# Opening of an attention-to-MLP kernel rewritten: four tiles transposed on TensorE, k-v moved behind the first MLP products, one excursion per tile

## The chip, the cores and the metric

One NeuronCore of one Trainium2 chip. The metric is the device time of one execution in microseconds; lower is better.

## The reference

A gated linear attention (r, k, v: 4 x 8 heads x 768 x 48), its output as 3072 rows of 384 features, and two MLPs behind it, all in float32.

```python
for t in range(S):
    kt, vt, rt = k[:, :, t], v[:, :, t], r[:, :, t]
    cur = einsum('bhd,bhe->bhde', u[None] * kt, vt)
    y[:, :, t] = einsum('bhd,bhde->bhe', rt, state + cur)
    state = w[None, :, :, None] * state + einsum('bhd,bhe->bhde', kt, vt)
h = x @ w_in;  g = relu(h) ** 2;     x = g @ w_out      # 384 -> 2048 -> 384
h = x @ w_in2; g = h - tanh(h);      x = g @ w_out2
```

## The kernel before

The sequence is cut into chunks of 128 positions; 4 batches x 6 chunks are 24 tiles, four tiles (TPB, one chunk of each batch) make a block of 512 rows, six blocks. A tile is loaded twice: "tt" holds r and k transposed (features on partitions), "nat" holds r, k, v with positions on partitions. Its steps: `decay` (DVE, L741) multiplies tt by powers of w; `products` (GpSimd, L316, L318) forms r k u, `bonus` (DVE, L747) sums it to one number per head, `diagonal` (ACT, L399) writes these as diagonal matrices; `score` (TensorE, L569) makes kT x rT, `mask` (DVE, L754) copies the causal half beside the diagonal; `attend` (TensorE, L583 for the state, L597 for v) makes the output, `x_high` (ACT, L407) and `x_low` (DVE, L780) split it into two fp32r parts; `decay_k` (GpSimd, L324) and the k-v product (TensorE, L605, the end of `attend`) feed `update_state` (DVE, L769 to L775).

The MLPs run in 96 steps each, m = 16 i + n: `first1(m)` is 9 products of 512 columns into hid, `act1` (DVE, L788, L790), `hi1` (ACT, L413) and `lo1` (GpSimd, L329) make the two parts of g, `second1(m)` is 9 products into acc. `first1` runs LAG = 3 steps ahead. Weights come in eight units per MLP; each is split by `split_hi` (ACT, L392) and `split_lo` (DVE, L799, or GpSimd, L335, for units 0 and 1). The raw units of MLP 1 lie in four stages that share their space with tiles; SP loads them in a written order (L260 to L282).

All engines run an order written out by hand, each waiting on counting semaphores. Tile T of blocks 1 to 5 is scored at n = 0, 3, 6, 9 of the block before and attended one step later (`scores_at`, `y_at`); `prepare_at` has its decay and bonus one step ahead of the scores. `stay_warm` multiplies the identity with itself. The second MLP has `poly_pick` (L847 to L858) in place of `act1`; its last three steps take the low part of g last (`second2_low_last`, L662, L663, L666).

## Time and profile before

| | us |
|---|---|
| median of 3 runs | 921.73 (920.44 to 923.01) |
| the profiled execution | 922.49 |
| its span, first to last instruction | 920.7 |

| stretch, us | PE busy | DVE busy | granted clock | DMA GB/s |
|---|---|---|---|---|
| 0 to 10 | 8.34 | 7.20 | 1.00 | 294 |
| 10 to 20 | 4.97 | 5.15 | 0.83 | 291 |
| 20 to 30 | 5.23 | 5.16 | 0.66 | 200 |
| 30 to 40 | 6.98 | 4.45 | 0.66 | 2 |
| 40 to 50 | 9.32 | 3.22 | 1.00 | 205 |
| 50 to 60 | 6.93 | 8.18 | 0.97 | 312 |
| 60 to 70 | 10.00 | 4.34 | 0.86 | 2 |
| 200 to 300 | 100.00 | 50.45 | 1.00 | 62 |

The first table tells the total, the second where TensorE is not filled. The granted clock is a share of full speed, so 0.5 is 1.2 GHz and 1.0 is 2.4 GHz; where TensorE stands, it says nothing of work. The first product of MLP 1 starts at 46 us.

### The profile page before, as it was taken

To read this page: it belongs to the slowest core of one execution; us is meant where nothing else is said; L and a number is where in the kernel's file an instruction comes from. 1 tells how busy PE (TensorE), PEld (TensorE's weight loads), DVE (VectorE), ACT (ScalarE), POOL (GpSimd) and SP (SyncE) were. 2 spreads that over 40 slices of the span, in tenths; PEclk is the share of its full clock that TensorE was granted. 3 is DMA by queue.
4 is the path that set the end of the run, shared out by engine and by line. 5 is a ranking of instruction groups with operands and counts; after the bars stand their busy time and mean duration, and the time that the engine had idled before them with its cause. 6 is when DMAs were issued, how large, how long until landed. Compare 5 with 4: busy or idle time off the path is not lost.

```text
span 920.7 us, 13868 instructions
## 1 busy us (share of the span) xinstructions
PE 896.6 (97%) x5340; PEld 736.9 (80%) x5340; DVE 591.2 (64%) x789; ACT 453.1 (49%) x852; POOL 477.1 (52%) x370
## 2 busy tenths in 40 slices
PE   5789999999999999999999999999999999999997
PEld 5668788888888888888888878888888888888886
DVE  6358736545563555445346668778787787787775
ACT  3333414222231322323124477777777777777774
POOL 5543434525443442433225776666666666666664
PEclk9799999999999999999999999999999999999999
DMA  6253111120311112020212200000000000000000
GB/s 254 107 206 140 53 54 54 58 103 1 106 54 54 53 54 106 1 92 16 103 35 69 68 1 1 35 1 1 34 1 1 35 1 0 36 1 1 35 0 35
DMA packets 12162, 47.49 MB, mean 52 GB/s; under 512 B 1472, under 2 KB 1600, under 8 KB 12096
## 3 DMA queue, kind: packets, MB, share of 16 engines
q1 hardware_dynamic: 12096, 46.60, 13.8%
q8 instruction: 42, 0.69, 0.3%
q14 instruction: 24, 0.20, 0.1%
HBM read 41.88 MB, written 4.72 MB: 51 GB/s over the span
## 4 chain that ended last, share of the span: by engine, by line
PE 82%; DVE 8%; POOL 4%; ACT 3%; issue 2%; DMA 1%; ACTq 0%; DVEq 0%; POOLq 0%
PE acc L551 13%; PE acc L553 12%; PE acc L552 12%; PE hid L551 9%; PE hid L552 9%; PE hid L553 9%; PE sc L552 3%; PE sc L553 3%; PE sc L551 3%; PE sc L569 2%; PE y L597 2%; PE sc L605 2%; PE y L583 2%; POOL area L340 1%; DVE area L847 1%
## 5 line engine op out<-in xcount | busy, mean ns | idle before, releaser
L329 POOL TENSOR_TENSOR g_l<-g_f,g_h 128x512 fp32r<-128x512 f32 x96 | 131.6, 1372 | 278.1 <-ACT g_h L413 278.1
L551 PE MATMUL acc<-g_h,wout_h 128*128 128x512 f32 x567 | 225.8, 398 | 0.6 <-POOL g_l L345 0.5
L553 PE MATMUL acc<-g_h,wout_l 128*128 128x512 f32 x567 | 221.9, 391 | 0.0
L552 PE MATMUL acc<-g_l,wout_h 128*128 128x512 f32 x567 | 221.4, 391 | 0.0
L413 ACT ACTIVATE g_h<-g_f 128x512 fp32r<-128x512 f32 x96 | 60.7, 632 | 315.8 <-DVE g_f L790 299.4
L340 POOL TENSOR_TENSOR area<-area 128x512 f32<-128x512 f32 x96 | 125.8, 1311 | 104.6 <-ACT area L431 104.6
L788 DVE TENSOR_SCALAR g_f<-hid 128x512 f32<-128x512 f32 x96 | 66.2, 690 | 164.4 <-PE hid L553 161.5
L551 PE MATMUL hid<-x_h,win_h 128*128 128x512 f32 x432 | 168.5, 390 | 1.2 <-DVE g_f L788 1.2
L552 PE MATMUL hid<-x_l,win_h 128*128 128x512 f32 x432 | 168.1, 389 | 0.0
L553 PE MATMUL hid<-x_h,win_l 128*128 128x512 f32 x432 | 168.0, 389 | 0.0
L345 POOL TENSOR_TENSOR g_l<-g_f,g_h 128x512 fp32r<-128x512 f32 x96 | 128.4, 1338 | 33.6 <-ACT g_h L446 33.6
L551 PEld LDWEIGHTS acc<-g_h,wout_h 128*128 128x128 f32 x567 | 106.7, 188 | 25.8 <-POOL g_l L345 1.5
L847 DVE TENSOR_SCALAR area<-area 128x512 f32<-128x512 f32 x96 | 88.3, 920 | 59.3 <-POOL area L340 59.3
L553 PEld LDWEIGHTS acc<-g_h,wout_l 128*128 128x128 f32 x567 | 106.8, 188 | 22.8
L552 PEld LDWEIGHTS acc<-g_l,wout_h 128*128 128x128 f32 x567 | 106.8, 188 | 21.0
L551 PEld LDWEIGHTS hid<-x_h,win_h 128*128 128x128 f32 x432 | 81.2, 188 | 18.7 <-DVE g_f L788 1.8
L553 PEld LDWEIGHTS hid<-x_h,win_l 128*128 128x128 f32 x432 | 81.1, 188 | 17.0
L552 PEld LDWEIGHTS hid<-x_l,win_h 128*128 128x128 f32 x432 | 81.2, 188 | 16.9
L853 DVE COPY_PREDICATED area<-area,y 128x512 f32<-128x512 uint32 x96 | 71.7, 747 | 3.3
L790 DVE TENSOR_TENSOR g_f<-g_f 128x512 f32<-128x512 f32 x96 | 70.9, 738 | 3.3
L399 ACT ACTIVATE area<-area,x2T 128x128 f32<-128x128 f32 x192 | 58.8, 389 | 28.8 <-DVE x2T L747 28.8
L439 ACT ACTIVATE area<-area 128x512 f32<-128x512 f32 x96 | 60.0, 625 | 19.4 <-POOL area L340 19.4
(110 smaller groups left out, 1169.7 us busy)
## 6 DMA issues: line engine op xcount, KB each, us to landing
x2T<-in_nat SPq DMA_DIRECT2D x13, 672.0 KB, 5.8
area<-in_nat SPq DMA_DIRECT2D x11, 672.0 KB, 4.9
x2T<-in_tt SPq DMA_DIRECT2D x12, 512.0 KB, 3.8
area<-in_tt SPq DMA_DIRECT2D x11, 512.0 KB, 3.6
out<-x2T SPq DMA_DIRECT2D x18, 256.0 KB, 2.2
x2T<-in_win SPq DMA_DIRECT2D x4, 768.0 KB, 7.7
x2T<-in_wout SPq DMA_DIRECT2D x4, 768.0 KB, 5.0
area<-in_win SPq DMA_DIRECT2D x4, 768.0 KB, 4.4
```

The source lines that it names most:

```text
L329: pool.tensor_tensor(g_l[:, m % 4, :], g_f[:, m % 2, :], g_h[:, m % 4, :].bitcast(F32), ALU.subtract).then_inc(s_gl1, 1)
L340: pool.tensor_tensor(ratio[m % 2], ratio[m % 2], sq[m % 2], ALU.mult).then_inc(s_pp, 1)
L345: pool.tensor_tensor(g_l[:, m % 4, :], g_f[:, m % 2, :], g_h[:, m % 4, :].bitcast(F32), ALU.subtract).then_inc(s_gl2, 1)
L413: act.activation(g_h[:, m % 4, :], g_f[:, m % 2, :], ACT.Copy).then_inc(s_gh1, 1)
L439: act.activation(ratio[m % 2], ratio[m % 2], ACT.Copy, scale=C5, bias=1.0).then_inc(s_ratio, 1)
L551: pe.matmul(dst, wh, xh, start=first, stop=False)
L552: pe.matmul(dst, wh, xl, start=False, stop=False)
L553: return pe.matmul(dst, wl, xh, start=False, stop=last)
L788: dve.tensor_scalar(g, hid1[m % 2], 0.0, None, ALU.max).then_inc(s_relu, 1)
L790: dve.tensor_tensor(g, g, g, ALU.mult).then_inc(s_g1, 1)
L847: dve.tensor_scalar(sq[m % 2], sq[m % 2], Q_SMALL, None, ALU.is_ge).then_inc(s_big, 1)
L853: dve.copy_predicated(tanh[m % 2], sq[m % 2].bitcast(U32), tanh_ps[:, :]).then_inc(s_sel, 1)
```

## The change

Tiles 0 to 3 come as nat alone; TensorE transposes their r and k (`transposed`), and DVE multiplies the result by the powers out of PSUM, in two halves. GpSimd does the four tiles' products first and then the whole split of unit 0, high part too. The powers of w are made with fewer waits, partly on ACT. K-v leaves `attend`: `key_value` runs behind attend(3) for tiles 0 and 2 and behind first1(0) for 1 and 3, as 16 products of 32 rows and 48 columns. The fillers are spread over the opening. From block 0 on, score(T + 1), attend(T) and key_value(T) stand together at n = 1, 4, 7, 10, score(4) alone at m = 0; decay and bonus of tile T + 2 follow one step later, and key_value(T) waits for mask(T + 1), whose scores share its bank. SP loads tiles 4 and 5 ahead of units 3 to 7 and tiles 6 and on behind them. Channel order in the weights is the natural one. At the end, first2(95) follows first2(94), and four steps take the low part last. Cut to its core, eight blanks of indentation less:

```diff
-NATW = C + H * HP + PAIRS * VW
-WARM_UP = 24
+RK = H * HP
+NATW = 2 * RK + PAIRS * VW
+WARM_UP = 6
...
+def prod_of(T):
+    if T < TPB:
+        return first_prod[:, C * (T % 2):C * (T % 2) + C].rearrange("p (h d) -> p h d", h=H)
+    return r_of(T)
...
+def decays(T):
+    return 2 * (T + 1) if T < TPB else TPB + T + 1
+KV_FIRST = [0, 2, 1, 3]
+def kv_count(T):
+    return KV_FIRST.index(T) + 1 if T < TPB else T + 1
+def kv_ps(T):
+    at = 512 * (T // 2) if T < TPB else 0
+    return sc_ps(T)[:, at:at + PAIRS * D]
...
+def slot_at(i, n):
+    return TPB * (i + 1) + n // 3 if 0 <= i < BLOCKS - 1 and n % 3 == 1 and 0 <= n < 12 else None
+def update_at(i, n):
+    return slot_at(i, n - 1)
+def diagonal_at(i, n):
+    T = slot_at(i, n + 1)
+    return T + 1 if T is not None and T + 1 < TILES else None
+def decay_k_at(i, n):
+    return slot_at(i, n + 1)
 def prepare_at(i, n):
-    if n == FT - 1:
-        return scores_at(i + 1, 0)
-    return scores_at(i, n + 1)
-def products_at(i, n):
-    if n >= FT - 2:
-        return scores_at(i + 1, 0) if n == FT - 2 else None
-    return scores_at(i, n + 2)
+    T = slot_at(i, n - 1)
+    if i == 0 and n == 0:
+        return TPB + 1
+    return T + 2 if T is not None and T + 2 < TILES else None
...
-        if n in (1, 5, 6, 7):
-            sp.wait_ge(*lo_done(0, {1: 0, 5: 1, 6: 2, 7: 3}[n]))
+        if n in (4, 5):
+            sp.wait_ge(s_kv, TPB)
+        elif n >= 2:
+            sp.wait_ge(*lo_done(0, {2: 0, 3: 1, 6: 2, 7: 3}[n]))
         at = STAGE1_AT[n]
         sp.dma_start(stage1[at], (wout1 if n % 2 else win1)[n // 2]).then_inc(s_stage1[at], 16)
     def load_tile(T):
-        before = T - 2 if T > 5 else T - 4
-        if before < LAST_KV:
-            sp.wait_ge(s_kv, before + 1)
+        before = T - 2
+        if before < TPB:
+            sp.wait_ge(s_sc, before + 1)
         else:
             sp.wait_ge(s_y, before + 1)
         load_tt(T)
+        if T < TPB + 2:
+            sp.wait_ge(s_kv, kv_count(T - TPB))
+        elif before < LAST_KV:
+            sp.wait_ge(s_kv, kv_count(before))
         load_nat(T)
...
-    load_tt(0)
     load_nat(0)
     sp.dma_start(u_all, u_rep).then_inc(s_u, 16)
-    load_tt(1)
-    load_nat(1)
+    for T in range(1, TPB):
+        load_nat(T)
     load_unit1(0)
-    load_nat(2)
-    load_tt(2)
-    load_nat(3)
-    load_tt(3)
     load_unit1(1)
-    load_tile(4)
-    sp.wait_ge(s_kv, TPB)
     load_unit1(2)
-    load_unit1(3)
-    load_unit1(4)
-    load_tile(5)
-    load_unit1(5)
-    load_unit1(6)
-    load_unit1(7)
+    load_tile(TPB)
+    load_tile(TPB + 1)
+    for n in range(3, UNITS):
+        load_unit1(n)
     for T in range(6, TILES):
         load_tile(T)
...
+    pool.memset(state_all, 0.0).then_inc(s_const, 1)
...
+        prod = prod_of(T)
+        if T < TPB:
+            after(pool, s_c, T - 1)
+        pool.tensor_tensor(prod, r, k, ALU.mult).then_inc(s_rk, 1)
         pool.wait_ge(s_rk, T + 1)
-        pool.tensor_tensor(r, r, u_all, ALU.mult).then_inc(s_ruk, 1)
+        pool.tensor_tensor(prod, prod, u_all.rearrange("p (h d) -> p h d", h=H), ALU.mult).then_inc(s_ruk, 1)
...
+        if T < TPB:
+            pool.wait_ge(s_tr, 2 * T + 2)
...
+    for T in range(TPB):
+        products(T)
+    pool.wait_ge(*landed(0, 0))
+    pool.tensor_copy(unit_parts(0)[0], unit_raw(0, 0)).then_inc(s_whi0, 1)
+    split_lo(0, 0)
     pool.wait_ge(s_tab, 1)
-    decay_k(0)
-    products(1)
-    decay_k(1)
-    split_lo(0, 0)
-    for T in range(2, TPB):
-        products(T)
-        decay_k(T)
+    decay_k(KV_FIRST[0])
+    decay_k(KV_FIRST[1])
+    decay_k(KV_FIRST[2])
+    decay_k(KV_FIRST[3])
     split_lo(0, 1)
...
-            T = prepare_at(i, n)
+            T = decay_k_at(i, n)
             if T is not None:
                 decay_k(T)
-            if i == 0 and n == 0:
-                decay_k(TPB)
-            T = products_at(i, n)
...
+    half = P // 2
+    act.wait_ge(s_setup, 14)
+    act.activation(pow_k[:, :, 0:half], pow_r[:, :, P - 1:half - 1:-1], ACT.Copy).then_inc(s_pow, 1)
+    act.wait_ge(s_setup, SETUP_DONE)
+    act.activation(pow_k[:, :, half:P], pow_r[:, :, half - 1::-1], ACT.Copy).then_inc(s_pow, 1)
+    for side in range(2):
+        rows = slice(HP * side, HP * side + D)
+        act.activation(dec_tile[rows, :, D * side:D * side + D],
+                       w_pow[rows, 7, :].unsqueeze(2).to_broadcast([D, PAIRS, D]), ACT.Copy).then_inc(s_tile, 1)
     act.wait_ge(s_powT, 1)
-    act.activation(dec_k, hid34[:, 0:512].rearrange("p (h e) -> p h e", h=H)[:, :, 0:D],
-                   ACT.Copy).then_inc(s_tab, 1)
+    act.activation(dec_k, acc2[:, :].rearrange("p (h e) -> p h e", h=H)[:, :, 0:D], ACT.Copy).then_inc(s_tab, 1)
     act.wait_ge(s_const, 3)
     diagonal(0)
     diagonal(1)
-    split_hi(0, 0)
+    diagonal(2)
     x_high(0)
-    diagonal(2)
+    diagonal(3)
     x_high(1)
-    diagonal(3)
     x_high(2)
+    x_high(3)
     split_hi(0, 1)
-    x_high(3)
     split_hi(0, 2)
...
+            if m == 0:
+                diagonal(TPB)
+            T = diagonal_at(i, n)
             if T is not None:
                 diagonal(T)
             if m + LAG < STEPS:
                 hi1(m + LAG)
-            T = y_at(i, n)
+            T = slot_at(i, n)
             if T is not None:
                 x_high(T)
...
-    def stay_warm(count):
+    def stay_warm(count, bank):
         for _ in range(count):
-            pe.matmul(hid34[:, 512:512 + P], ident, ident, start=True, stop=True)
+            pe.matmul(bank[:, 0:P], ident, ident, start=True, stop=True)
+    def transposed(T):
+        pe.wait_ge(s_nat[set_of(T)], 16)
+        rk = set_nat[set_of(T)][:, 0:2 * RK]
+        for half in range(2):
+            after(pe, s_dec, 2 * (T - 1) + half + 1)
+            for a in range(PAIRS):
+                at = 512 * half + P * a
+                mm = pe.transpose(hid34[:, at:at + P], rk[:, at:at + P], ident)
+            mm.then_inc(s_tr, 1)
     def score(T):
-        pe.wait_ge(s_dec, T + 1)
-        before = T - 1 if T < TPB else T
-        after(pe, s_scm, before)
-        after(pe, s_state, min(before, LAST_KV))
+        pe.wait_ge(s_dec, decays(T))
+        after(pe, s_scm, T - 1 if T < TPB else T)
+        if T >= TPB:
+            pe.wait_ge(s_state, min(T if T == TPB else T - 1, LAST_KV))
         rT, kT, dst = rT_of(T), kT_of(T), sc_ps(T)
         for a in range(PAIRS):
             for g in range(2):
         opened = [False] * 4
         after(pe, s_xl, T - 1 if T < TPB else T)
         if T >= TPB:
-            pe.wait_ge(s_state, T - 3)
+            pe.wait_ge(s_state, kv_count(T - TPB))
             for a in range(PAIRS):
                 for part in range(3):
                     c, quad = divmod(3 * a + part, 4)
         turns = [[], [], [], []]
         for a in range(PAIRS):
-            for part, at, head in ((0, 0, 0), (1, 32, 1), (2, 64, 0), (2, 80, 1)):
+            for part, at, head in ((0, 0, 0), (1, 32, 0), (1, 48, 1), (2, 80, 1)):
                 c, quad = divmod(3 * a + part, 4)
                 turns[quad].append((a, c, at, head))
         for turn in range(4):
                                skip_group_check=True)
                 opened[quad] = True
         mm.then_inc(s_y, 1)
-        if T < LAST_KV:
-            pe.wait_ge(s_kd, T + 1)
-            for a in range(PAIRS):
-                mm = pe.matmul(sc_ps(T)[:, VW * a:VW * a + VW], k_of(T)[:, P * a:P * a + P], v[:, a, :],
-                               start=True, stop=True)
-            mm.then_inc(s_kv, 1)
+    def key_value(T):
+        if T >= LAST_KV:
+            return
+        pe.wait_ge(s_scm, T + 1 if T < TPB else T + 2)
+        pe.wait_ge(s_kd, kv_count(T))
+        for a in range(PAIRS):
+            for quad in range(4):
+                at = HP * (quad // 2)
+                mm = pe.matmul(kv_ps(T)[32 * quad:32 * quad + 32, D * a:D * a + D],
+                               k_of(T)[:, P * a + 32 * quad:P * a + 32 * quad + 32],
+                               v_of(T)[:, a, at:at + D], start=True, stop=True)
+        mm.then_inc(s_kv, 1)
...
-    stay_warm(WARM_UP)
+    stay_warm(WARM_UP, hid34)
+    transposed(0)
+    stay_warm(4, y7)
     pe.wait_ge(s_pow, 2)
     for a in range(PAIRS):
-        mm = pe.transpose(hid34[:, P * a:P * a + P], pow_k[:, a, :], ident)
+        mm = pe.transpose(acc2[:, P * a:P * a + P], pow_k[:, a, :], ident)
     mm.then_inc(s_powT, 1)
+    stay_warm(4, y7)
     score(0)
+    transposed(1)
+    stay_warm(8, y7)
     score(1)
+    transposed(2)
+    stay_warm(8, y7)
+    transposed(3)
+    stay_warm(8, y7)
     attend(0)
     score(2)
+    pe.wait_ge(s_tab, 1)
+    stay_warm(8, acc2)
     attend(1)
     score(3)
+    stay_warm(8, hid34)
     attend(2)
-    stay_warm(8)
+    stay_warm(8, hid34)
     attend(3)
-    stay_warm(12)
+    key_value(KV_FIRST[0])
+    key_value(KV_FIRST[1])
     for m in range(LAG):
         first1(m)
+        if m == 0:
+            key_value(KV_FIRST[2])
+            key_value(KV_FIRST[3])
     for i in range(BLOCKS):
         for n in range(FT):
             m = FT * i + n
                 first1(m + LAG)
             else:
                 first2(m + LAG - STEPS)
-            if scores_at(i, n) is not None:
-                score(scores_at(i, n))
-            if y_at(i, n) is not None:
-                attend(y_at(i, n))
+            T = slot_at(i, n)
+            if m == 0:
+                score(TPB)
+            if T is not None:
+                if T + 1 < TILES:
+                    score(T + 1)
+                attend(T)
+                key_value(T)
             second1(m)
     for m in range(STEPS):
-        if m + LAG < STEPS:
+        if m + LAG < STEPS - 1:
             first2(m + LAG)
+            if m + LAG == STEPS - 2:
+                first2(STEPS - 1)
+        if m + LAG < STEPS - 1:
             second2(m)
         else:
             second2_low_last(m)
...
     def decay(T):
-        dve.wait_ge(s_tt[set_of(T)], 16 * loads_of(T))
-        both = set_tt[set_of(T)]
-        dve.tensor_tensor(both, both, dec_tt, ALU.mult).then_inc(s_dec, 1)
+        if T >= TPB:
+            dve.wait_ge(s_tt[T % 2], 16 * tt_loads(T))
+            dve.tensor_tensor(set_tt[T % 2], set_tt[T % 2], dec_tt, ALU.mult).then_inc(s_dec, 1)
+            return
+        after(dve, s_sc, T - 1)
+        for half in range(2):
+            at = slice(512 * half, 512 * half + 512)
+            dve.wait_ge(s_tr, 2 * T + half + 1)
+            if T == 0 and half == 1:
+                dve.wait_ge(s_pow, 2)
+            dve.tensor_tensor(set_tt[T % 2][:, at], hid34[:, at], dec_tt[:, at], ALU.mult).then_inc(s_dec, 1)
...
         dve.wait_ge(s_ruk, T + 1)
         after(dve, s_diag, T - 1)
-        dve.tensor_reduce(c_sum[T % 2], r_of(T).rearrange("p (h d) -> p h d", h=H), AX_X,
-                          ALU.add).then_inc(s_c, 1)
+        dve.tensor_reduce(c_sum[T % 2], prod_of(T), AX_X, ALU.add).then_inc(s_c, 1)
...
+        for g in range(2):
+            rows, cols = slice(HP * g, HP * g + HP), slice(D * g, D * g + D)
+            kv = kv_ps(T)[rows, :].rearrange("p (a e) -> p a e", a=PAIRS)
+            if T < TPB:
+                ins = dve.tensor_tensor(st[rows, :, cols], kv, dec_tile[rows, :, cols], ALU.mult)
+            else:
+                ins = dve.tensor_tensor(st[rows, :, cols], kv, st[rows, :, cols], ALU.add)
+            ins.then_inc(s_state if T < TPB and g == 1 else s_sum, 1)
...
+    half = P // 2
+    dve.memset(dec_tile, 0.0).then_inc(s_setup, 1)
+    dve.memset(pow_r[:, :, half:half + 1], 1.0).then_inc(s_setup, 1)
     dve.wait_ge(s_w, 16)
-    for i in range(7):
-        link(dve.tensor_tensor(w_pow[:, i + 1, :], w_pow[:, i, :], w_pow[:, i, :], ALU.mult))
-    link(dve.reciprocal(pow_r[:, :, 0], w_pow[:, 6, :]))
-    for i in range(7):
+    for i in range(6):
         e = 1 << i
-        step = w_pow[:, i, :].unsqueeze(2).to_broadcast([P, PAIRS, e])
-        link(dve.tensor_tensor(pow_r[:, :, e:2 * e], pow_r[:, :, 0:e], step, ALU.mult))
-    dve.tensor_copy(pow_k, pow_r[:, :, ::-1]).then_inc(s_pow, 2)
-    dve.wait_ge(s_pow, 2)
+        dve.wait_ge(s_setup, 2 * i + 2)
+        dve.tensor_tensor(pow_r[:, :, half + e:half + 2 * e], pow_r[:, :, half:half + e],
+                          w_pow[:, i, :].unsqueeze(2).to_broadcast([P, PAIRS, e]),
+                          ALU.mult).then_inc(s_setup, 1)
+        squared(i)
+    dve.wait_ge(s_setup, 14)
+    dve.reciprocal(w_pow[:, 8, :], w_pow[:, 6, :]).then_inc(s_setup, 1)
+    squared(6)
+    dve.wait_ge(s_setup, 16)
+    dve.tensor_tensor(pow_r[:, :, 0:half], pow_r[:, :, half:P],
+                      w_pow[:, 8, :].unsqueeze(2).to_broadcast([P, PAIRS, half]), ALU.mult).then_inc(s_setup, 1)
+    dve.wait_ge(s_setup, SETUP_DONE)
     decay(0)
-    for side, at, width in ((0, 0, 32), (1, 32, 32), (0, 64, 16), (1, 80, 16)):
-        rows = slice(HP * side, HP * side + D)
-        link(dve.tensor_copy(dec_tile[rows, :, at:at + width],
-                             w_pow[rows, 7, :].unsqueeze(2).to_broadcast([D, PAIRS, width])))
-    dve.wait_ge(s_const, 4)
     bonus(0)
     decay(1)
-    mask(0)
     bonus(1)
-    update_state(0)
-    x_low(0)
-    mask(1)
     decay(2)
     bonus(2)
-    update_state(1)
+    dve.wait_ge(s_const, 4)
+    mask(0)
+    bonus(3)
+    decay(3)
+    mask(1)
+    x_low(0)
+    mask(2)
     x_low(1)
-    mask(2)
-    decay(3)
-    bonus(3)
-    update_state(2)
+    mask(3)
     x_low(2)
-    mask(3)
-    update_state(3)
     x_low(3)
+    dve.wait_ge(s_const, 5)
+    update_state(KV_FIRST[0])
+    act1(0)
+    update_state(KV_FIRST[1])
+    update_state(KV_FIRST[2])
+    act1(1)
+    update_state(KV_FIRST[3])
+    act1(2)
     split_lo(0, 2)
-    for m in range(LAG):
-        act1(m)
     decay(TPB)
     bonus(TPB)
...
-            T = x_low_at(i, n)
+            T = update_at(i, n)
+            if T is not None:
+                update_state(T)
+            T = slot_at(i, n)
+            if T is not None and T + 1 < TILES:
+                mask(T + 1)
+            if m + LAG < STEPS:
+                act1(m + LAG)
+            if m == 0:
+                mask(TPB)
             if T is not None:
                 x_low(T)
-                update_state(T)
-            if m + LAG < STEPS:
-                act1(m + LAG)
-            T = scores_at(i, n)
-            if T is not None:
-                mask(T)
             T = prepare_at(i, n)
             if T is not None:
                 decay(T)
```

## Rows read from the trace of the kernel before

**Rows 1.** The page, part 1: engine busy us (share of the span) xinstructions.
```profile
PE 896.6 (97%) x5340; PEld 736.9 (80%) x5340; DVE 591.2 (64%) x789; ACT 453.1 (49%) x852; POOL 477.1 (52%) x370
```

**Rows 2.** Timeline, one tile in the steady state: start, us, engine, line, what.
```profile
157.78 0.39 PE L553 MATMUL hid<-x_h,win_l 128*128 128x512 f32 x1
...
158.10 0.97 PEld L569 LDWEIGHTS sc<-area 64*128 64x128 f32 x16 [0.35 <-issue]
...
159.53 0.39 PE L552 MATMUL acc<-g_l,wout_h 128*128 128x512 f32 x1
...
163.19 0.39 PE L553 MATMUL hid<-x_h,win_l 128*128 128x512 f32 x1
...
163.50 0.59 PEld L583 LDWEIGHTS y<-area 128*32 128x32 f32 x24 [0.35 <-issue]
...
165.17 0.97 PEld L605 LDWEIGHTS sc<-area 128*128 128x128 f32 x8 [0.20 <-issue]
...
166.40 0.39 PE L552 MATMUL acc<-g_l,wout_h 128*128 128x512 f32 x1
```

**Rows 3.** Timeline of TensorE in the opening.
```profile
1.66 7.09 PE L558 MATMUL hid<-area 128*128 128x128 f32 x48 [1.66 <-POOL area L305]
...
24.32 1.78 PEld L569 LDWEIGHTS sc<-x2T 64*128 64x128 f32 x16 [5.53 <-DVE x2T L741]
...
43.36 2.76 PEld L558 LDWEIGHTS hid<-area 128*128 128x128 f32 x24
...
46.06 0.48 PE L551 MATMUL hid<-x_h,win_h 128*128 128x512 f32 x1
```

**Rows 4.** Windows: us; busy PE, PEld, DVE, ACT, POOL; granted clock; DMA share, GB/s.
```profile
24.00:26.00 2.00, 1.68 (x16) 1.68 (x16) 0.26 (x1) 0.00 (x0) 1.92 (x2) 0.50 0.88 246
...
60.00:61.00 1.00, 1.00 (x4) 0.71 (x4) 0.61 (x2) 1.00 (x4) 0.00 (x0) 0.50 0.00 0
```

**Rows 5.** Timeline of TensorE behind the opening.
```profile
57.88 0.97 PEld L569 LDWEIGHTS sc<-x2T 64*128 64x128 f32 x16 [2.33 <-DVE x2T L741]
```

**Rows 6.** Timeline, first GpSimd product and first decay.
```profile
6.47 1.23 DVE L741 TENSOR_TENSOR x2T<-x2T,area 128x1024 f32<-128x1024 f32 x1
...
7.15 1.40 POOL L316 TENSOR_TENSOR x2T<-x2T 128x384 f32<-128x384 f32 x1 [5.30 <-DMA area<-in_u_rep]
```

**Rows 7.** Timeline of SP, and the DMA view of 70 to 80 us (us to landing).
```profile
71.07 0.33 SPq L249 DMA_DIRECT2D x2T<-in_wout  x1
...
71.92 0.43 SPq L243 DMA_DIRECT2D x2T<-in_nat  x1
...
x2T<-in_nat SPq DMA_DIRECT2D x1, 672.0 KB, 6.4
```

**Rows 8.** Timeline of 57 to 69 us: steps of a tile and of a unit.
```profile
57.74 0.55 DVE L747 TENSOR_REDUCE x2T<-x2T 128x8 f32<-128x384 f32 x1
...
58.32 2.45 ACT L399 ACTIVATE area<-area,x2T 128x128 f32<-128x128 f32 x8 [0.97 <-DVE x2T L747]
...
60.87 1.34 DVE L754 COPY_PREDICATED area<-x2T,sc 128x1024 f32<-128x1024 uint32 x1 [0.39 <-ACT area L399]
...
66.98 0.47 ACT L407 ACTIVATE x_h<-y 128x384 fp32r<-128x384 f32 x1
...
67.35 1.48 ACT L392 ACTIVATE wout_h<-x2T 128x1536 fp32r<-128x1536 f32 x1
...
68.86 2.18 DVE L799 TENSOR_TENSOR wout_l<-x2T,wout_h 128x1536 fp32r<-128x1536 f32 x1 [2.45 <-ACT wout_h L392]
```

**Rows 9.** The page, part 5: busy us, mean ns of one, idle before.
```profile
L788 DVE TENSOR_SCALAR g_f<-hid 128x512 f32<-128x512 f32 x96 | 66.2, 690 | 164.4 <-PE hid L553 161.5
...
L413 ACT ACTIVATE g_h<-g_f 128x512 fp32r<-128x512 f32 x96 | 60.7, 632 | 315.8 <-DVE g_f L790 299.4
```

**Rows 10.** Line L318 by source: duration ns min/median/max.
```profile
L318 POOL TENSOR_TENSOR x2T<-x2T,area x13: 995/1005/2400, 8.6 to 407.1; 128x384 f32<-128x384 f32 x13
```

**Rows 11.** Timeline of TensorE, last step.
```profile
914.37 0.50 PE L662 MATMUL acc<-g_h,wout_h 128*128 128x512 f32 x1 [0.90 <-ACT g_h L446]
```

103 lines of the change are left out of this document (40 added, 63 removed).

## The prediction

> **What bounds the kernel now.** I read the page first [rows 1]: TensorE is busy for 97% of the span, so outside the opening only work taken off TensorE, or a wait of TensorE removed, can move the time. The steady state is seen in the timeline of one tile [rows 2]: the matrix products follow each other every 0.227 us, 18 to a step, 4.09 us. Into this stream come two excursions per tile. The scores delay it from the product at 157.78 to the second one at 159.53: 1.75 less two intervals of 0.227, 1.30 us. Attention and k-v delay it from 163.19 to 166.40: 2.76 us. Together 4.05 us for a tile.
>
> The opening is different. The first MLP product starts at 46.04 us [rows 3]; up to there TensorE mostly waits for DVE or runs at half clock: the 16 score instructions that load in 0.97 us at 158.10 [rows 2] take 1.78 us at 24.32 [rows 3], and the clock view has 0.50 there [rows 4]. After 46 us TensorE loses little: 1.9 us (the weight loads 2.33) ahead of 57.88 on the decay of tile 4 [rows 5], and part of 59 to 63 us, where the granted clock is 0.50 (1.2 of 2.4 GHz) although the engine is busy [rows 4]; what it did before is that wait for tile 4 and a shorter one ahead of it. The change therefore has 46 us of opening to win from, some 5 us of stalls behind it, and 20 pairs of excursions.
>
> **The new opening.** The four 512 KB tile loads of transposed r and k go, so the natural tile 0 comes first. The old u_rep landed at 7.1 us [rows 6] with 1.36 MB queued up to and with it; three loads of 1.95 MB land 7.2 us after the issue of the first (71.07 to 71.92 plus 6.4) [rows 7]. By the slope between the two, about 0.45 MB per us, 0.75 MB issued at 1.2 us land near 5.5 us. From there TensorE has a nearly gapless list. Fillers: 56, at 2.76 us for 12 [rows 3], 12.9 us. Transposes, not in the old trace but for four: 36, 0.115 us each by the rows of the same 128-column shape, 4.2 us (from below half of it, from above 0.21 at half clock). Scores: 4 x 1.09 [rows 2]. Attention: 4 x 1.1, from the part of 163.50 to 165.17 that has no state product. K-v of two tiles: 1.9 us. Sum 27.7 us. The old start took 7.09 us for 24 fillers against 5.5 at the later rate [rows 3], so a cold start costs 1.6 us; I add 1.7. The first MLP product comes at F = 35.0 us, 11 us earlier. DVE's chain beside this list is shorter: from attend(1) to attend(3) it is a diagonal 2.45, x_high 0.47, x_low 0.55, mask 1.34 [rows 8], 4.9 us, against 5.9 us of TensorE's list; the two multiplies of a half tile are hidden behind fillers. The DVE set-up, whose last step gave way to decay(0) at 6.47 us [rows 6], has fewer waits between its steps and part of it moves to ACT; I take it under tile 0's landing and transposes. GpSimd has the four products (8 us), the new copy of unit 0 (estimate 1.7 us as half of a two-input 3.4, up to 3.5), its low part and four decays: done by about 27 us, under the 33 at which k-v wants them. The state memset lies under the wait for DMA. If that cover goes, each us is a us of F. Bounds for F: 33.5 (no cold part) to 38.
>
> **Behind the opening: what is late next.** I follow the written order of each engine, in us after F. TensorE: first1(0) 2.05, k-v of tiles 1 and 3 1.9, first1(1) and (2) 4.1, done at 8.2. DVE now puts act1(2) (0.69 + 0.7 [rows 9]) ahead of split_lo(0,2) (2.18) and that ahead of decay(4) (1.23) [rows 6, 8]: decay(4) ends at 13.0, while TensorE, after first1(3), wants it at 10.2. Stall 2.9, where the old one was 1.9. Then tile 4 and tile 5 are prepared one after the other, each a bonus 0.55, a diagonal 2.45, a mask 1.34 and between them a decay 1.23 [rows 6, 8]: mask(5) ends at 23.1.
>
> Here the new wait bites: key_value(T) writes the bank in which score(T+1) has just been put, so it waits for mask(T+1), and second1 and everything behind it queue behind that wait. For tile 4 TensorE stands 1.9 us. For tile 5 it is worse. SP has units 3 to 7 ahead of the loads of tile 6, and unit 7 waits for split_lo(0,3). That ends after mask(5) by act1(4) 1.4, hi1 0.65, x_high 0.45, split_hi(0,3) 1.48 and split_lo 2.18 [rows 8, 9]: at 29.2. Unit 7, tt 6 and nat 6 then land 7.4 us later [rows 7], at 36.6. The old order needed tile 6 only at step 5; the new one needs it at step 2. GpSimd's products 2.1 [rows 10] (38.7), bonus 0.6, diagonal 2.45, hi1(6) 0.65, split_hi(0,4) 1.45, split_lo(0,4) 2.2, which DVE has ahead of the mask, and mask(6) 1.4 end at 47.5. TensorE has 16.1 us of work from mask(5) on (k-v, three second1, three first1, score(6), attend(5)) and stands at 39.2. Stall 8.3 us. Whatever else TensorE loses before it is absorbed by it.
>
> From F + 47.5 to the start of the second block's steps I count k-v 1.0, second1 2.05, 11 steps of 4.09 and two excursions of 3.81: 55.7 us; the clock that falls in so long a wait costs 2 us more (the part of 59 to 63 us at half clock [rows 4], some 3.4 us, cost 1.7). Units 4 to 7 and tiles 7 and 8 come in time in this count, unit 6 by 1 us only. Sum 35.0 + 47.5 + 57.7 = 140.2 us. The old trace has 139.6 there (the score at 141.75 less a first1 of 2.05 and the gap). So the 11 us of opening are given back, +0.6.
>
> **The merged excursion.** From the last product to the score load 0.32, score 1.09 with its drain, attention 1.47, k-v, switch 0.20, re-entry 0.34, less 0.454 [rows 2]: 2.96 + k-v. K-v becomes 32 instructions with 48 columns instead of 8 with 112. None such is in the trace. The nearest are L583, 24 of the same tile shape in 0.59 us, 24.6 ns each, and the old k-v, 8 in 0.97, 0.12 us each. By columns alone (48 for 112) it could be 0.4, by the old row 0.97; I take 0.85, between L583's pitch (0.79) and the old row. That makes 3.81, 0.24 less than 4.05; even at 0.4 it would be 0.7 less. The wait for mask(T+1) takes some back: score's end 1.20 after its load, mask 1.37, hand-over 0.1, so 2.66, against attention's end at 2.56, and the re-entry after a wait 0.1. Left: 0.1 per tile with k-v, between -0.3 and 0.5. For tiles 8 to 19 it is 1.2 us, for 20 to 22, without k-v, 0.2 each, 0.6. Score(8) has already been done in block 0: 1.3.
> The row shows 24.6 ns with 128 columns in four column tiles. The Trainium skill, "TensorE: Matmul & The Clock Gate", section "Wait — 56ns, not 53.3ns?", says that start-to-start doesn't fall below about 25 ns however few the columns. By that 48 columns would gain nothing over 128: k-v 0.8, not 0.4, and the excursion stays near my value.
>
> **The tail.** first2(95) moves ahead of second2(91) and one more step takes its low part last. TensorE's last wait, 0.9 us at 914.37 on ACT's g_h [rows 11], goes: with the hidden product 2 us earlier, the chain of poly and pick ends under second2's products. -1.0, between -1.3 and +0.3.
>
> **Sum.** 920.7 + 0.6 - 1.2 - 0.6 - 1.3 - 1.0 = 917.2 us of span, 3.5 less; the profiled execution took 922.49 with 920.7 of span, the median of the runs is 921.73, and I apply the difference to that: 918.2 us. 0.3%, about what a measurement can tell from no change here, is 2.8 us, so the border to "faster" is 918.96.
>
> **Rivals.**
> (A) The 8.3 us stall doesn't come, because tile 6 lands or is masked in time. Against it stand the SP order and the split_lo in front of the mask. It would give 918.2 - 8.3 - 2 = 907.9. Chance 0.15.
> (B) The chain to mask(6) is longer than my minimum durations: one GpSimd product has 2.40 us against 1.0 [rows 10], and DVE and GpSimd work side by side here. 3 to 4 us more on it go one to one into the time: 921.7, no change. Chance 0.20.
> (C) Slower. The half clock stays through the opening. The old half clock at 24.32 followed a wait of TensorE of 5.5 us [rows 3, 4]; the new opening fills such gaps, but 36 of its instructions are transposes, whose effect on the clock no row shows. If they don't hold it, 16 us of the list at half clock bring 8 us more: F = 43 and 926.2 us. It decides from 13 us of half clock on (6.3 us more, over 924.5). Chance 0.12.
> The Trainium skill, "TensorE: Matmul & The Clock Gate", section "Part 4: PE-mode transpose", states that transpose mode doesn't engage the full clock in the way that a matmul does; that is the rule by which (C) would come out.
> The forecast itself has 0.53. Its own range is 914.5 to 922.5: F -1.5/+3, chain 2, excursions 2 to 3, tail 1, not all at once. It lies below 918.96 with some six tenths of its weight. Faster: 0.53 x 0.62 + 0.15, with a little for a shorter stall, 0.50. Slower 0.12 + 0.01. Same 0.37. The range, 911 to 925, leaves out most of (A) and (C).
>
> **What would show it.** First MLP product at 33.5 to 38 us. TensorE idle 2 to 3 us ahead of score(4), about 2 ahead of the k-v of tile 4, and 6 to 10 us ahead of that of tile 5, released by DVE's mask, with the nat 6 load landing some 37 us after F. Granted clock 1.00 through most of 10 to 35 us. Excursions of 3.8 to 4.0 us for score, attention and k-v together, k-v loads of 0.8 to 0.9. No wait on ACT's g_h in the last step. Wrong it would be if the second block began well before 136 us (A), or if k-v waited for the mask by more than 0.3 us in every tile, which over 15 tiles costs 4 us.

## The result, and the profile after

The changed kernel takes 909.63 us (median of 4 runs, 908.87 to 911.24) against 921.60 (4 runs, 920.44 to 923.01): a ratio of 0.9872, with the interval 0.9852 to 0.9891. It is faster by 12.0 us. The forecast was 918.2, and 909.63 lies below its range. The profiled execution took 909.35 us with a span of 907.4, where before had 920.7; 13.3 us of span are to be placed.

The page first, part 1 and the row of granted clock in part 2 (the latter in 40 slices of 22.7 us, tenths of full speed):

```profile
PE 886.2 (98%) x5888; PEld 733.9 (81%) x5888; DVE 596.4 (66%) x789; ACT 451.6 (50%) x855; POOL 490.6 (54%) x372
...
PEclk9987999999999999999999999999999999999999
```

TensorE is busy for 886.2 us instead of 896.6 [rows 1]. Of the 13.3 us, 10.4 are time in which it worked: work that it no longer does, or does in less time. The forecast gave the excursions only 3.1 us. The two slices below 9 in the clock row (45 to 91 us) are places to look at for waits.

The opening, in the timeline of TensorE (start, us, engine, line, what; in brackets the idle time before it and who ended it), and the windows over it (busy PE, PEld, DVE, ACT, POOL; granted clock; DMA share, GB/s):

```profile
5.65 0.85 PEld L610 LDWEIGHTS hid<-area,x2T 128*128 128x128 f32 x8 [1.35 <-DMA x2T<-in_nat]
...
32.81 0.50 PE L593 MATMUL hid<-x_h,win_h 128*128 128x512 f32 x1 [0.51 <-DVE x_l L863]
```

```profile
10.00:30.00 20.00, 20.00 (x263) 18.56 (x262) 11.72 (x16) 9.97 (x32) 13.39 (x11) 1.00 0.45 164
```

Tile 0 loads its first transposes at 5.65 us (5.5 was forecast), TensorE is busy without a gap from 10 to 30 us at granted clock 1.00, where the old opening had 0.50 at 24 us [rows 4], and the first MLP product comes at 32.81 us against 46.06 [rows 3]. So the opening alone is 13.2 us shorter.

What comes behind it, in the timeline of DVE, GpSimd and TensorE around the scores of tile 4:

```profile
45.61 2.28 DVE L817 TENSOR_TENSOR x2T<-x2T,area 128x1024 f32<-128x1024 f32 x1
...
46.77 1.98 POOL L355 TENSOR_TENSOR x2T<-x2T,area 128x384 f32<-128x384 f32 x1
...
47.94 2.08 PE L622 MATMUL sc<-x2T 64*128 64x128 f32 x16 [5.63 <-DVE x2T L817]
```

TensorE waits 5.63 us for decay(4). Before, the same wait was 1.91 us on the product (2.33 on the weight load [rows 5]), and 2.9 was forecast. The granted clock behind it is 0.50 from 48 to 52 us. Then the chain to mask(6), in the timeline of SP, GpSimd, DVE, ACT and TensorE from 63 to 82 us, and the windows behind it:

```profile
63.78 0.33 SPq L280 DMA_DIRECT2D x2T<-in_wout  x1
...
64.63 0.44 SPq L272 DMA_DIRECT2D x2T<-in_nat  x1
...
71.14 1.00 POOL L345 TENSOR_TENSOR x2T<-x2T 128x384 f32<-128x384 f32 x1 [9.55 <-DMA x2T<-in_nat]
...
73.86 2.45 ACT L432 ACTIVATE area<-area,x2T 128x128 f32<-128x128 f32 x8 [6.74 <-DVE x2T L831]
...
76.73 1.47 ACT L425 ACTIVATE win_h<-x2T 128x1536 fp32r<-128x1536 f32 x1
...
78.23 1.76 DVE L882 TENSOR_TENSOR win_l<-x2T,win_h 128x1536 fp32r<-128x1536 f32 x1 [2.26 <-ACT win_h L425]
79.91 1.28 DVE L837 COPY_PREDICATED area<-x2T,sc 128x1024 f32<-128x1024 uint32 x1
...
81.24 0.68 PEld L664 LDWEIGHTS sc<-area 128*32 128x32 f32 x32 [7.40 <-DVE area L837]
81.25 0.87 PE L664 MATMUL sc<-area 128*32 128x48 f32 x32 [7.13 <-DVE area L837]
```

```profile
81.00:85.00 4.00, 3.75 (x39) 3.06 (x40) 2.07 (x5) 2.38 (x3) 1.29 (x1) 0.50 0.45 132
85.00:88.00 3.00, 3.00 (x10) 2.35 (x10) 2.93 (x4) 0.00 (x0) 1.75 (x2) 0.65 0.18 75
88.00:92.00 4.00, 4.00 (x19) 3.31 (x18) 2.98 (x4) 0.77 (x2) 1.91 (x2) 1.00 0.02 4
```

This is the forecast chain link by link. SP sends unit 7 only when split_lo(0,3) is done, tile 6's nat behind it lands 6.5 us later and lets GpSimd begin at 71.14; bonus, diagonal, split_hi, split_lo and mask follow, and k-v of tile 5, which has to wait for mask(6), starts at 81.25 after TensorE has stood for 7.13 us. The clock is then 0.50 (1.2 GHz) up to 87 us, where the products come 0.43 us apart instead of 0.23, and 1.00 from 88.

The steady state, one tile, in the timeline of TensorE and DVE (the first line is the first product of the second block's steps):

```profile
138.88 0.39 PE L593 MATMUL hid<-x_h,win_h 128*128 128x512 f32 x1
...
144.78 0.39 PE L595 MATMUL hid<-x_h,win_l 128*128 128x512 f32 x1
145.09 0.97 PEld L622 LDWEIGHTS sc<-area 64*128 64x128 f32 x16 [0.35 <-issue]
...
146.30 1.36 DVE L837 COPY_PREDICATED area<-x2T,sc 128x1024 f32<-128x1024 uint32 x1 [3.76 <-PE sc L622]
146.76 0.89 PEld L650 LDWEIGHTS y<-area,x2T 128*32 128x32 f32 x32
...
147.72 0.41 PEld L664 LDWEIGHTS sc<-x2T 128*32 128x32 f32 x32
...
148.20 0.19 PEld L593 LDWEIGHTS acc<-g_h,wout_h 128*128 128x128 f32 x1
...
148.54 0.39 PE L594 MATMUL acc<-g_l,wout_h 128*128 128x512 f32 x1
...
160.67 1.16 PE L622 MATMUL sc<-x2T 64*128 64x128 f32 x16
```

These rows answer to [rows 2]. From the product at 144.78 to the second one behind the excursion at 148.54 are 3.76 us, less two intervals of 0.227: 3.31 us, where before had 4.05 in two parts. K-v's 32 instructions load in 0.41 us, and from its start to the next weight load at 148.20 are 0.48 us. DVE's mask ends at 147.66, and k-v starts at 147.72. Ahead of the second block one more k-v waits for its mask, that of tile 7, by 0.54 us at 115.81; behind it none does by more than 0.3 us. The period of a tile, 145.09 to 160.67, is 15.58 us; before it was 174.46 less 158.10, 16.36 (the next scores in the old trace start at 174.46). That is 0.78 us per tile.

The end, in the timeline of TensorE, the first product of each of the last two steps:

```profile
899.15 0.39 PE L722 MATMUL acc<-g_h,wout_h 128*128 128x512 f32 x1
...
901.19 0.39 PE L722 MATMUL acc<-g_h,wout_h 128*128 128x512 f32 x1
```

They stand 2.04 us apart and the last doesn't wait, where before the last one waited 0.90 us [rows 11].

The account, by the two places where the traces can be laid over each other. The steps of the second block start at 138.88 us against 139.61: 0.7 us earlier, although the opening had won 13.2. From there to the end of the span it is 768.5 us against 781.1: 12.6 us. Of these, twelve tiles at 0.78 are 9.4; 1.1 is the tail; 1.3 is the score of tile 8, which is now done in the first block and so is moved, not saved. Tiles 20 to 22 have no k-v: their scores stand 15.22 us apart (381.06, 396.28, 411.50), where the old trace has 15.47 (402.49, 417.96, 433.42), which makes 0.8. Sum 12.6. So nearly all that the change brings comes from the excursions, and the opening, for which most of the diff was written, brings almost nothing.

### The profile page after: what moved, and what is told of

Its sections match the earlier page's. It is cut to its first block, busy times and chain, and to the rows that moved or that the text cites. A ratio compares the mean times of both kernels' runs of the same rounds, so it can differ in the third digit from the quotient of the medians.

```text
span 907.4 us, 14993 instructions
## 1 busy us (share of the span) xinstructions
PE 886.2 (98%) x5888; PEld 733.9 (81%) x5888; DVE 596.4 (66%) x789; ACT 451.6 (50%) x855; POOL 490.6 (54%) x372
## 4 chain that ended last, share of the span: by engine, by line
PE 89%; DVE 4%; ACT 2%; POOL 2%; issue 1%; DMA 1%; SPq 0%; ACTq 0%; DVEq 0%; POOLq 0%
PE acc L593 14%; PE acc L594 13%; PE acc L595 13%; PE hid L593 10%; PE hid L594 10%; PE hid L595 10%; PE sc L594 3%; PE sc L593 3%; PE sc L595 3%; PE sc L622 3%; PE y L650 2%; PE y L636 1%; DMA x2T<-in_nat 1%; PE y L600 1%; POOL wout_l L369 1%
## 5 line engine op out<-in xcount | busy, mean ns | idle before, releaser
L873 DVE TENSOR_TENSOR g_f<-g_f 128x512 f32<-128x512 f32 x96 | 80.3, 837 | 3.3
```

What stands on the lines that cost most here:

```text
L873: dve.tensor_tensor(g, g, g, ALU.mult).then_inc(s_g1, 1)
```

## Experiments

Two theories stood against each other. Theory 1: k-v by 32 columns is much cheaper than the 0.85 us that I took, by columns rather than by instructions, and this carries the gain; the opening is given back to the wait for mask(6). Its rival: the gain is that of the merged excursion, or of the opening, and k-v's price isn't what counts. Each run below is the changed kernel with the edit shown; "over" and "under" are against its median of 909.63.

One thing is needed to read them. The opening itself doesn't take the same time in every execution (more under the hardware, below), and the four to ten runs of one kernel lie 1.3 to 3.2 us apart, in one case 4.7. A difference of one or two microseconds between two medians can be that. The traces separate it, since they show when the first MLP product starts (F), when the steps of the second block start, and what is left from there:

| trace | F | second block | between | to the end |
|---|---|---|---|---|
| before | 46.06 | 139.61 | 93.6 | 781.1 |
| changed | 32.81 | 138.88 | 106.1 | 768.5 |
| k-v wide | 33.45 | 139.58 | 106.1 | 774.9 |
| excursion apart | 32.79 | 136.48 | 103.7 | 771.9 |
| both undone | 36.01 | 141.07 | 105.1 | 778.5 |
| tile 6 early | 34.38 | 131.62 | 97.2 | 768.5 |
| tile 4 early | 35.21 | 138.64 | 103.4 | 768.5 |
| both, with split_lo moved | 34.81 | 131.73 | 96.9 | 768.6 |
| both, without that move | 34.71 | 130.07 | 95.4 | 768.7 |
| without 48 fillers | 31.19 | 137.18 | 106.0 | 768.5 |
| both early, without 48 fillers | 30.20 | 125.92 | 95.7 | 768.7 |
| old tail | 35.18 | 140.56 | 105.4 | 769.7 |

**K-v again as 4 products of 128 rows and 112 columns a tile, all else as changed.**

```diff
-for quad in range(4):
-    mm = pe.matmul(kv_ps(T)[32 * quad:32 * quad + 32, D * a:D * a + D], k_of(T)[:, P * a + 32 * quad:...], ...)
+mm = pe.matmul(kv_ps(T)[:, VW * a:VW * a + VW], k_of(T)[:, P * a:P * a + P], v_of(T)[:, a, :], ...)
```

> The changed kernel with one thing undone: k-v again as 4 products of 128 rows and 112 columns per tile in place of 16 of 32 rows and 48 columns. In the changed kernel's trace the 32 short instructions load in 0.41 us and the way back to the MLP product is 0.07 us, against 0.97 and 0.20 (inside the 1.09) in the old form. Theory 1 (my forecast missed because it priced k-v at 0.85 us plus a switch of 0.20): each tile from 6 to 19 costs 0.6 us more, 14 tiles 8.5 us, and the four k-v of the opening some 2 us, since the wait of tile 5 hangs on them: 8 to 11 us over the changed kernel, 918 to 920.5 us. Rival 2 (the gain is that of standing in one excursion, whatever k-v's form): not over 3 us, under 913 us.

Measured: 917.50 us (6 runs, 916.50 to 919.49), 0.9956 [0.9943, 0.9969]. It is 7.9 over. Its steady excursion, in the timeline of TensorE:

```profile
161.59 0.39 PE L595 MATMUL hid<-x_h,win_l 128*128 128x512 f32 x1
...
163.57 0.89 PEld L650 LDWEIGHTS y<-area 128*32 128x32 f32 x32
...
164.67 0.97 PEld L662 LDWEIGHTS sc<-area 128*128 128x128 f32 x8 [0.20 <-DVE area L834]
...
165.58 0.48 PE L593 MATMUL acc<-g_h,wout_h 128*128 128x512 f32 x1
...
165.90 0.39 PE L594 MATMUL acc<-g_l,wout_h 128*128 128x512 f32 x1
```

From 161.59 to 165.90 less 0.454 it is 3.86 us, 0.55 more than 3.31. K-v to the next product takes 0.91 instead of 0.48, and its start comes 1.10 us behind the start of L650's loads instead of 0.96. The row names the mask as what it waited for, but the old trace has the same 1.10 at that place (164.07 to 165.17), where k-v waits for no mask: going from column tiles of 32 into a whole array takes 0.14 us that the short form doesn't pay there. Twelve tiles at 0.54 (scores 16.12 us apart instead of 15.58) are the 6.4 us by which the trace is longer from the second block on; only 0.7 stands ahead of it, in F, so what the wide k-v of tiles 4 to 7 costs is hidden by the waits there. 917.50 is a little under the range that Theory 1 gave, which had counted 2 us for the opening. Theory 1 stands in its mechanism and the rival without k-v falls.

**The excursion taken apart: score(T + 1) ahead of second1, attend and k-v behind it; k-v by 32 columns.**

```diff
         score(T + 1)
+second1(m)
+if T is not None:
     attend(T)
     key_value(T)
-second1(m)
```

> The changed kernel with the excursion cut in two: score(T+1) stays ahead of second1, attend(T) and key_value(T) go behind it. Short k-v is kept. Theory 1 (a second break costs what the old rows show, 0.08 + 0.1 + a drain, 0.2 to 0.3 us): 17 tiles, 3.5 to 5 us more, less up to 2 us, because second1(4) now lies under the wait of k-v of tile 5: 911 to 914 us. Rival 2 (one excursion carries most of the 12 us gained behind block 0): 917 us or more.

Measured: 911.76 us (4 runs, 910.38 to 913.53), 0.9892 [0.9874, 0.9910], 2.1 over. By the rows of its trace the excursions delay the MLP by 1.30 + 2.20 = 3.50 us per tile against 3.31, and its scores stand 15.80 us apart instead of 15.58. From the second block on it is 3.4 us longer. It takes 2.4 of them back ahead of it: the stall at the k-v of tile 5 is 5.34 us instead of 7.13, since a second1 now stands ahead of it. So the merge is worth more in the steady state than the 2.1 us of the medians, and it makes the stall longer.

**Both undone, with the new opening, order of loads and tail.**

```diff
-for quad in range(4):
-    mm = pe.matmul(kv_ps(T)[32 * quad:...], ...)
+mm = pe.matmul(kv_ps(T)[:, VW * a:VW * a + VW], ...)
...
         score(T + 1)
+second1(m)
+if T is not None:
     attend(T)
     key_value(T)
-second1(m)
```

> Wide k-v and excursion cut in two together, so that of the change the new opening, the order of loads and preparations, and the tail remain. Theory 1: 10 to 14 us over the changed kernel, within 2 us of the kernel before (919.5 to 923.5): the opening's 13 us are given back in block 0. Rival (the opening keeps several us of its gain): under 917 us.

Measured: 920.34 us (10 runs, 918.85 to 921.74), 0.9988 [0.9977, 0.9998]. The rows: where its MLP starts, and the two waits behind it.

```profile
36.01 0.48 PE L593 MATMUL hid<-x_h,win_h 128*128 128x512 f32 x1
...
50.60 1.65 PE L622 MATMUL sc<-x2T 64*128 64x128 f32 x12 [4.35 <-DVE x2T L815]
...
84.56 2.05 PE L662 MATMUL sc<-area 128*128 128x112 f32 x8 [4.86 <-DVE area L835]
```

10 us won in the opening (46.06 to 36.01) leave 1.4 us at the end (the median of the kernel before beside it is 921.72), and the tail is among them. Its second block starts at 141.07 us, 1.5 later than in the old trace, with the 1.3 us of tile 8's score already done: by the traces the new opening and the order behind it win nothing. The four variants form a square: split and long 920.34, merged and long 917.50, split and short 911.76, merged and short 909.63. K-v's form is worth 8.6 or 7.9, the merge 2.8 or 2.1, and they add up. From the second block on the traces say the same with less scatter: k-v's form 6.6 or 6.4, the merge 3.6 or 3.4.

**SP loads tile 6 ahead of unit 7.**

```diff
-for n in range(3, UNITS):
+for n in range(3, UNITS - 1):
     load_unit1(n)
-for T in range(6, TILES):
+load_tile(6)
+load_unit1(UNITS - 1)
+for T in range(7, TILES):
```

> The changed kernel with one line of SP moved: the loads of tile 6 are issued ahead of unit 7 instead of behind it, so they wait for k-v of tile 4 (59 us) and no longer for the split of unit 3 (63.8 us). Theory (the 7.1 us that TensorE stands ahead of k-v of tile 5 is the chain unit 7's wait, landing of nat 6, products, bonus, diagonal, split, mask): bonus(6) comes some 5 us earlier, the stall falls to 1 to 2.5 us and the half clock behind it goes too, 6 to 8 us less, 902 to 904 us. Rival (something else is late next: unit 7, which lands later, at second1(12), or DVE's split of unit 4): under 3 us gained, over 906.5 us.

Measured: 902.87 us (4 runs, 902.07 to 904.36), 0.9803 [0.9787, 0.9819], 6.8 under. The k-v of tile 5 in its timeline:

```profile
76.86 0.55 PE L666 MATMUL sc<-area 128*32 128x48 f32 x32 [1.65 <-DVE area L839]
```

It waits 1.65 us instead of 7.13, and the granted clock is 1.00 from 70 to 86 us. Moving one load in the written order of SP returns 6.8 us of the opening that the same order had eaten; that the stall came from this order is thereby shown. Between F and the second block the trace has 97.2 us instead of 106.1, 8.8 less: 5.5 of wait and the rest mostly half clock. The new order had made this stretch 12.5 us longer than in the old trace, so this one load is about seven tenths of it. What is left holds the wait for tile 4, 3.7 us longer than before with half clock behind it, and the score of tile 8, less what the shorter excursions win.

**Tile 4 prepared earlier: its decay ahead of act1(0), its bonus ahead of act1(2).**

```diff
 update_state(KV_FIRST[0])
+decay(TPB)
 act1(0)
...
 act1(1)
+bonus(TPB)
 update_state(KV_FIRST[3])
 act1(2)
 split_lo(0, 2)
-decay(TPB)
-bonus(TPB)
```

> The changed kernel with DVE's order behind the opening altered: decay(4) ahead of act1(0), bonus(4) ahead of act1(2), split_lo of unit 2 last. Theory (TensorE's 5.6 us ahead of score(4) and the half clock behind it are on the chain to mask(6), which has no slack of its own): mask(5) and all behind it come 4 to 6 us earlier, 903.5 to 905.5 us. Rival (the wait of k-v of tile 5 absorbs what is won, since its chain starts at a point that doesn't move): within 1.5 us of the changed kernel.

Measured: 908.75 us (4 runs, 906.07 to 909.10), 0.9855 [0.9834, 0.9877], 0.9 under. By the medians my theory fell and the rival held. The timeline of TensorE shows where the win went, and that this is half of the story:

```profile
46.01 1.16 PE L622 MATMUL sc<-x2T 64*128 64x128 f32 x16 [0.50 <-DVE area L852]
...
53.66 1.16 PE L622 MATMUL sc<-area 64*128 64x128 f32 x16 [2.19 <-DVE area L817]
...
59.02 0.55 PE L664 MATMUL sc<-x2T 128*32 128x48 f32 x32 [1.28 <-DVE area L837]
...
81.95 0.87 PE L664 MATMUL sc<-area 128*32 128x48 f32 x32 [7.14 <-DVE area L837]
```

The wait ahead of score(4) is 0.50 instead of 5.63. Of these 5.1 us, 2.19 come back ahead of score(5) and 1.28 ahead of the k-v of tile 4. The other 1.7 are won: the wait for mask(6) is as long as before (7.14 against 7.13), but the chain to it starts earlier too. Unit 7 is sent 29.3 us behind F instead of 31.0, the k-v of tile 5 starts 46.7 us behind F (35.21 in this trace) against 48.4, and the second block 103.4 against 106.1. That is 2.6 us less; the old-tail trace, which has the same late F, has 105.4, so it is 1.9 to 2.6. The rival's premise, a chain that starts at a point that doesn't move, is not what the trace shows; the win was hidden by an F that came 2.4 us later than in the changed kernel's trace.

**Both, and split_lo of unit 4 behind mask(6).**

```diff
-if i == 0 and SPLIT1_AT.get(n, 0) not in LO_POOL[0]:
+if i == 0 and n != 3 and SPLIT1_AT.get(n, 0) not in LO_POOL[0]:
+    if n == 4:
+        split_lo(0, 4)
     split_lo(0, SPLIT1_AT[n])
```

> Both of the last two, and split_lo of unit 4 behind mask(6) instead of ahead of it. Theory: both stalls (5.6 and 7.1 us) and the stretches of half clock behind them (some 3.5 us) are open to be won; 11 to 15 us less than the changed kernel, 895 to 899 us. Rival (k-v of tile 4 or 5 waits for another mask instead): 900 to 903 us.

Measured: 902.58 us (4 runs, 902.27 to 903.79), 0.9800 [0.9786, 0.9815]. No better than tile 6 alone: the theory of 895 to 899 fell and the rival held. The new wait is seen in the timeline:

```profile
77.03 2.09 DVE L884 TENSOR_TENSOR win_l<-x2T,win_h 128x1536 fp32r<-128x1536 f32 x1
...
79.26 0.47 PE L595 MATMUL hid<-x_h,win_h 128*128 128x512 f32 x1 [2.21 <-DVE win_l L884]
```

The split, moved behind the mask, is now late for first1(8), which waits 2.21 us for it.

**The same without that move of split_lo.**

```diff
+load_tile(6)
+load_unit1(UNITS - 1)
...
+decay(TPB)
 act1(0)
...
+bonus(TPB)
 update_state(KV_FIRST[3])
```

> Tile 6 loaded ahead of unit 7, and decay(4), bonus(4) ahead in DVE's order, but split_lo of unit 4 left at its place ahead of mask(6). In the run with all three, TensorE waited 2.2 us at first1(8) for unit 4's low part and 1.0 us ahead of k-v of tile 4. Theory (that 2.2 us was caused by my moving the split): it goes, and k-v of tile 5 waits 0 to 1 us instead: 0.5 to 2 us under that run's 902.6, 900.5 to 902 us. Rival (the split ahead of the mask costs as much there): 902.5 to 904 us.

Measured: 899.88 us (4 runs, 898.54 to 903.20), 0.9768 [0.9745, 0.9791], 2.7 less than with the move, and 3.0 less than with tile 6 alone, a little more than expected. The k-v of tile 5 waits 1.45 us. Between F and the second block the trace has 95.4 us against 97.2 with tile 6 alone. So the early preparation of tile 4 is worth 1.9 us here, and 1.9 to 2.6 with the long stall there: the 3.0 and 0.9 of the medians differ by the scatter of F and don't show that the stall had absorbed it.

**The 48 fillers in eights left out.**

```diff
 transposed(1)
-stay_warm(8, y7)
 score(1)
...
 transposed(3)
-stay_warm(8, y7)
 attend(0)
```

> The changed kernel without the 48 identity products that stand in eights between the pieces of the opening (those ahead of score(0) stay). Theory 1 (they only fill waits, and without them the granted clock falls to 0.5, as in the old opening): the first MLP product comes no earlier than 31 us and the time is within 3 us of the changed kernel on either side. Rival 2 (TensorE's list was the bound of the opening and the clock holds): 11 us of list go, DVE and ACT bound the opening at about 27 us, and 4 to 6 us are gained.

Measured: 906.59 us (4 runs, 905.05 to 907.76), 0.9840 [0.9823, 0.9858], 3.0 under. TensorE in the opening, and the windows with the clock:

```profile
25.15 1.08 PE L650 MATMUL y<-area,x2T 128*32 128x128 f32 x32 [0.88 <-DVE area L831]
...
28.05 1.94 PE L650 MATMUL acc<-area,x2T 128*32 128x128 f32 x32 [1.82 <-DVE area L831]
```

```profile
26.00:28.00 2.00, 0.23 (x11) 0.00 (x0) 1.85 (x3) 0.61 (x2) 0.00 (x0) 0.93 0.29 119
28.00:30.00 2.00, 1.95 (x45) 1.98 (x49) 0.34 (x1) 0.00 (x0) 0.00 (x0) 0.50 0.04 8
30.00:32.00 2.00, 2.00 (x68) 1.76 (x60) 1.18 (x3) 1.96 (x3) 0.01 (x1) 0.72 0.18 44
```

The 11 us of fillers stood mostly ahead of waits for DVE, four of them for its masks, which now show (1.03, 0.81, 0.88 and 1.82 us), and after the last one the clock is 0.50 from 28 to 31 us. The first MLP product comes at 31.19, 1.6 us earlier; against the traces whose first score starts as late as this one's (11.1 us; F 35.2) it is some 4. The stalls behind it (5.62 and 7.52 us) are as they were, and the stretch from F to the second block is the same (106.0 against 106.1): what the opening wins here goes into the time whole, and the chain behind it moves with F.

**Tile 6 early, tile 4 early, without the 48 fillers.**

```diff
+load_tile(6)
+load_unit1(UNITS - 1)
...
-stay_warm(8, y7)
...
+decay(TPB)
 act1(0)
```

> The last kernel without the 48 identity products in eights. Without them the changed kernel gained 3.0 us, its first MLP product at 31.2 us instead of 32.8 to 35.2, with 3 us at half clock just ahead of it. Theory (behind the opening the chains start at that product, so it carries over whole): 2 to 4 us less than the run beside it, 897.5 to 900 us. Rival (the half clock spreads, or the chain of decays and products that doesn't hang on TensorE binds now): within 1 us of the run beside it.

Measured: 896.38 us (4 runs, 895.96 to 897.48), 0.9726 [0.9710, 0.9742], a little under the expected range. It is the fastest of all, 25.7 us less than before (median 922.07 of the 7 runs beside it) and 13.3 under the changed kernel. Its windows have granted clock 1.00 from 20 to 34 us although the waits for the masks are there, 1.81 us the longest:

```profile
27.93 1.08 PE L652 MATMUL acc<-area,x2T 128*32 128x128 f32 x32 [1.81 <-DVE area L833]
...
30.20 0.49 PE L595 MATMUL hid<-x_h,win_h 128*128 128x512 f32 x1 [0.52 <-DVE x_l L859]
```

```profile
24.00:34.00 10.00, 6.79 (x208) 5.49 (x205) 6.87 (x10) 5.73 (x11) 4.58 (x3) 1.00 0.60 227
```

So with nearly the same wait the clock fell in one profiled execution and not in the other. What decides it isn't shown by these runs.

**The old tail.**

```diff
-if m + LAG < STEPS - 1:
+if m + LAG < STEPS:
     first2(m + LAG)
-    if m + LAG == STEPS - 2:
-        first2(STEPS - 1)
-if m + LAG < STEPS - 1:
     second2(m)
```

> The changed kernel with the end as before: first2(95) at its old place, three steps with the low part last. Theory: the old wait of 0.9 to 1.3 us on ACT's g_h in the last step comes back, 1.0 to 1.3 us more, 910.6 to 911. Rival: the early first2(95) costs as much elsewhere, no difference (within 0.4 us).

Measured: 912.19 us (4 runs, 911.13 to 912.42), 0.9893 [0.9876, 0.9909], 2.6 over.

The last two steps in its timeline of TensorE:

```profile
900.90 0.39 PE L722 MATMUL acc<-g_h,wout_h 128*128 128x512 f32 x1
...
904.00 0.50 PE L722 MATMUL acc<-g_h,wout_h 128*128 128x512 f32 x1 [0.90 <-ACT g_h L479]
```

The wait of 0.90 us on g_h is back as in [rows 11], and the last step comes 3.10 us behind the one before it instead of 2.04: 1.06 us for the tail. The other 1.5 us of the medians' difference isn't seen at the tail, and the median lies above the expected range by it. In this trace the first MLP product comes at 35.18 us instead of 32.81 with the same opening and the second block 1.7 us later; from there to the end it is 1.2 us longer. So 1.1 to 1.2 us are the tail, and the rest is the scatter of the opening.

**96 columns, and 24.** Each has the 32 instructions of the changed kernel with another number of columns, to see what sets their pitch.

```diff
-kv_ps(T)[32 * quad:32 * quad + 32, D * a:D * a + D], ..., v_of(T)[:, a, at:at + D]
+kv_ps(T)[32 * quad:32 * quad + 32, 96 * a:96 * a + 96], ..., v_of(T)[:, a, (at // 4):(at // 4) + 96]
```

> K-v with 96 columns instead of 48, the tile shape and count kept; the extra columns are not read. It measures what an instruction costs: 48 columns took 12.8 ns each (32 in 0.41 us). If the moving columns bound it, 96 take up to twice as long, 20 to 26 ns each, 0.65 to 0.82 us for a tile; if a floor of issue or weight load bounds it, 0.41 to 0.5.

```diff
-kv_ps(T)[32 * quad:32 * quad + 32, D * a:D * a + D], ..., v_of(T)[:, a, at:at + D]
+kv_ps(T)[32 * quad:32 * quad + 32, 24 * a:24 * a + 24], ..., v_of(T)[:, a, at:at + 24]
```

> K-v with 24 columns, so half of the state is left out and the output of blocks 1 to 5 is another. If columns bound the 12.8 ns, 24 take 6 to 8 ns, 0.2 to 0.26 us for a tile; if a floor does, the 0.41 stays.

Measured, one run each: 914.84 us and 908.0 us. The loads of k-v in the steady state, in the timeline of TensorE, with 96 columns first and then with 24:

```profile
149.39 0.65 PEld L664 LDWEIGHTS sc<-x2T 128*32 128x32 f32 x32
```

```profile
147.05 0.37 PEld L664 LDWEIGHTS sc<-x2T 128*32 128x32 f32 x32
```

In time per instruction: 24 columns 11.6 ns, 48 columns 12.8 (0.41 over 32), 96 columns 20.3, and the 128 columns of L650 0.89 over 32, 27.8 ns. 96 and 128 columns have nearly the same time per column, 0.21 and 0.22 ns, so up there the time goes by the columns. It does so with four tiles side by side: four instructions of 96 columns start in 81 ns, where one of 112 columns over the whole array took 121. From 48 to 24 columns the time hardly falls. What sets it there isn't shown; 24 columns neither kept the 0.41 us nor came down to 0.26, the two outcomes that had been named.

The distance from score to score says what k-v costs in all: 15.22 us without it (tiles 20 to 22), 15.53 with 24 columns, 15.58 with 48, 15.90 with 96, 16.12 in the wide form. So k-v takes 0.36 us of a tile as changed, and 0.90 in the wide form.

## Why the prediction was wrong

**The step that failed is the price of k-v by 32 columns.** I put it at 0.85 us between 0.4 and 0.97, "between L583's pitch (0.79) and the old row", with 0.20 for the way back. Measured are 0.48 for both together. The lower bound that I had worked out by columns was the right one, and I had chosen the row that it was nearest to by the tile's shape, not by what the pitch of that row depends on. L583 and L597 both have 128 columns; nothing in the old trace said that 24.6 ns was a floor and not a width. The Trainium skill's rule, "TensorE: Matmul & The Clock Gate", section "Wait — 56ns, not 53.3ns?", that start-to-start doesn't fall below some 25 ns, confirmed me in it; here 12.8 ns were measured, so the measurement decides: over four column tiles the rule doesn't hold. The Trainium skill's "TensorEngine Tiling (Array Packing)", section "Key Properties", says that different tiles can execute loads and products in parallel, and the rows agree with that (four instructions of 96 columns in 81 ns).

The mis-sized term spreads over the sum like this. Forecast 3.95 us per tile with the mask's share (3.81 + 0.14), measured 3.31. Of the 0.64, 0.57 is k-v with its way back (1.05 to 0.48) and 0.14 the wait and re-entry which isn't there; against them attention is 0.07 longer than 1.47, which holds the few hundredths that k-v does wait. Twelve tiles at 0.64 are 7.7 us of the 9.8 by which the forecast span of 917.2 is above 907.4; 1.3 are the start of the second block, below. The other 0.8 lie behind it too, where 777.0 us were forecast and 768.5 measured. By the distance from score to score a tile won 0.78, not the 0.74 between 4.05 and 3.31; with the forecast's 0.1, twelve tiles make 8.2 of these 8.5.

**The second block's start: right in its mechanism, 1.3 us too late.** 140.2 was forecast and 138.88 measured. F was 32.81 against 35.0: the 1.7 us for a slow start weren't there in this execution. But other kernels with the same opening had their first MLP product anywhere from 32.79 us (split excursion) to 34.38 (tile 6 early), 35.18 (old tail) and 35.21 (tile 4 early), so the 35.0 lay inside this scatter of 2.4 us, and the bound of 33.5 was a little too high. (The landing at 5.5 us was slightly misreckoned: the slope used gives 5.7, and 5.65 was measured.) F + 47.5 became F + 48.4. Unit 7 was sent at F + 31.0 (forecast 29.2), GpSimd began at F + 38.3 (36.6), and the rest took 10.0 us against 10.9 (split_lo 1.76 instead of 2.18). From the k-v of tile 5 to the second block it took 57.6 us; 57.7 was forecast, but this agreement is luck. With tile 6 early, at full clock, the same stretch took 54.8 us, so the half clock cost some 2.9 and not 2.0, and the work in it was 0.9 shorter than the 55.7 counted.

**Stalls.** Tile 5: 8.3 forecast, 7.13 measured. Tile 4's score: 2.9 forecast, 5.63 measured, since on DVE work beside GpSimd took longer than its row in the old trace: decay(4) 2.28 instead of 1.23, and the squares of act1 up to 1.76 instead of 0.7. Priced at their minimum durations, the chain was 2.1 us short (decay(4) ends at F + 15.1, not 13.0). The forecast said that whatever TensorE loses ahead of the larger stall is absorbed by it. The run with tile 4 early shows that this was half right: of 5.1 us of wait taken away, 1.9 to 2.6 reached the second block. The k-v of tile 4 was to wait 1.9 us; in the trace mask(5) ends at 58.25 and k-v starts at 58.30, 0.98 us behind the start of L650's loads where a tile of the steady state has 0.96: no wait, since TensorE came to it later by then.

**The merge and the mask.** The forecast let mask(T + 1) end 0.1 behind attention in every tile. It ends 0.06 before k-v starts. The merge, 0.24 less the wait, is 0.19 by the excursions and 0.22 by the distance of the scores.

**The tail.** 1.0 forecast, 1.06 measured.

**The rivals.** (A), no stall, would have been 907.9, close to the result, but it isn't what happened: the stall is there in the trace with 7.13 us, and taking it away gives another 6.8. A time that agrees with a rival is no evidence for it. (B), a longer chain, happened at tile 4 (decay(4) 2.1 us late), and part of it went into the time; the chain to mask(6) was only 0.9 longer than forecast. (C), half clock in the opening, didn't: 1.00 from 10 to 30 us with 36 transposes among the other instructions. The rule of the Trainium skill on which (C) leant ("TensorE: Matmul & The Clock Gate", "Part 4: PE-mode transpose") isn't refuted, since no run here had its transposes alone. The nearest is the run without the 48 fillers, where 16 transposes (tiles 2 and 3, 15.34 to 18.1 us) follow each other with no identity products between them, behind scores and ahead of attention: the granted clock was 1.00 from 14 to 26 us.

The chances: "faster" had 0.50, and the case that came in, the sum with a cheap k-v, had been worked out to 0.7 less per tile and then hardly entered the range, which allowed the excursions 2 to 3 us together. K-v at 0.4 instead of 0.85 over fifteen tiles is 6.8 us: 918.2 less 6.8 is 911.4 by this term alone, at the edge of the range.

## What to carry to other kernels

When an operation's form is absent from the trace and a bound by its size is far below the bound by the nearest row, keep the low bound in the range with the full number of times that it occurs, and ask whether the row's pitch is a floor or only the width of that row. Products in four column tiles were paid by their columns down to 96, and by some 12 ns each at 48, so 32 narrow ones were cheaper than 8 wide ones. And before shortening an opening, follow the load order behind it: here 13 us won in the opening were lost again before the second block, 8.8 by the traces to one transfer queued behind a late one, and moving that load ahead returned 6.8. Lastly, split a time at places that every variant has before comparing medians that are close: the same edit had 0.9 us in one pair of medians and 3.0 in another, and about 2 in both pairs of traces.

## What was unexpected of the hardware

- Instructions in four column tiles of 128 x 32 started every 12.8 ns with 48 columns, 11.6 with 24, 20.3 with 96, 27.8 with 128.
- A DVE multiply of two operands from SBUF, 128 x 1024, took 2.28 us at 45.61 while GpSimd worked on tensors too. Of the 20 decays of tiles 4 to 23 in this trace (L817), eleven began while a GpSimd tensor operation was running and took 2.05 to 2.28 us; the nine that began while none was took 1.20 to 1.23. Where GpSimd began second, its operation was the longer one (1.54 us instead of 1.28 at 90.98; its multiply of 128 x 384, 1.00 us alone, took 1.98 at 46.77). The Trainium skill, "GPSIMD Engine Reference", section "1. Specifications", says that GpSimd shares its SBUF interfaces with VectorE, with contention when a DVE instruction has two SBUF inputs; the rows agree.
- The same opening ended anywhere from 32.8 to 35.2 us. The difference arises in the first 10 us: tile 0's transposes, loaded in 0.85 us in the changed kernel's trace, take 1.57 in that of tile 4 early, and the next products are slow in the same measure, until the first score starts at 11.3 us instead of 8.9. The clock row shows 1.00 in both, so it doesn't tell these two cases apart; what does stays open. In thirteen traces the first score started at 8.9 to 9.0 us four times and at 10.5 to 11.6 nine times.

```profile
5.65 1.57 PEld L610 LDWEIGHTS hid<-area,x2T 128*128 128x128 f32 x8 [1.35 <-DMA x2T<-in_nat]
```

- After a wait of 7.13 us TensorE worked at half clock for nearly 6 us, to 87 us; after 1.65 us (tile 6 early) it didn't fall, and after 1.8 us in the opening it fell in one trace and not in another.
